# Attention probabilities transposed by the DMA engines as 16-bit planes instead of by TensorE

## The reference

```python
scores = scale * np.matmul(q_c, k_c.transpose(0, 1, 2, 4, 3))
scores = scores - np.max(scores, axis=-1, keepdims=True)
attn = np.exp(scores)
attn = attn / (np.sum(attn, axis=-1, keepdims=True) + 1e-09)
out = np.matmul(attn, v_c)
```

## Time and profile before

| | us |
|---|---|
| median of 3 runs (1153.63 to 1153.79) | 1153.75 |
| the profiled execution | 1154.12 |
| its span, first to last instruction | 1152.0 |
| PE busy | 1134.8 |
| ACT busy | 264.4 |
| DVE busy | 514.9 |

### The profile page before, as it was taken

The page is one execution under the profiler, slowest core; times in us unless marked ns, Lnnn a source line. Parts: engine busy times, 40 slices in busy tenths (PEclk is TensorE's granted clock), DMA queues, the critical chain, the costliest instruction groups (busy, mean ns, idle before and its releaser), DMA issues.

```text
span 1152.0 us, 19512 instructions
## 1 busy us (share of the span) xinstructions
PE 1134.8 (99%) x6790; PEld 998.3 (87%) x6791; DVE 514.9 (45%) x1142; ACT 264.4 (23%) x413; POOL 312.3 (27%) x191
## 2 busy tenths in 40 slices
PE   8999999999999999999999999999999999999995
PEld 5898889999999999999999998889987888888884
DVE  5454335222222222222223248888655555555553
ACT  3322232231111123111113211112333032032320
POOL 7300000060000006000002501100387686086680
PEclk8999999999999999999999999999999999999998
DMA  8221120330000012000002201101662662062630
GB/s 323 78 73 48 43 82 0 120 101 0 0 0 0 0 56 89 0 0 0 0 0 74 72 28 28 20 7 27 192 175 66 180 231 89 27 231 84 217 121 16
DMA packets 48881, 83.51 MB, mean 72 GB/s; under 512 B 8143, under 2 KB 32847, under 8 KB 48722
## 3 DMA queue, kind: packets, MB, share of 16 engines
q1 hardware_dynamic: 43922, 70.77, 19.4%
q0 software_dynamic: 4496, 11.56, 3.2%
q10 hardware_dynamic: 432, 0.79, 0.2%
HBM read 73.48 MB, written 10.92 MB: 73 GB/s over the span
## 4 chain that ended last, share of the span: by engine, by line
PE 98%; DMA 1%; DVE 0%; issue 0%; SPq 0%; ACT 0%; DVEq 0%
PE psum L1298 15%; PE psum L1300 15%; PE psum L1299 15%; PE psum L1332 12%; PE psum L1334 11%; PE psum L1333 11%; PE psum L1511 4%; PE psum L1513 4%; PE psum L1512 4%; PE psum L1495 2%; PE psum L1221 1%; PE psum L1472 1%; PE psum L1205 1%; PE psum L1213 1%; DMA qkT<-in_qk 1%; PE psum L1265 1%
## 5 line engine op out<-in xcount | busy, mean ns | idle before, releaser
L440 POOL TENSOR_TENSOR weights_r<-weights,weights_r 128x1024 fp32r<-128x1024 f32 x96 | 233.3, 2455 | 619.5 <-ACT weights_r L611 618.3
L1298 PE MATMUL psum<-xhi,weights_r 128*128 128x384 f32 x768 | 259.0, 337 | 0.3 <-DVEq L816 0.3
L1300 PE MATMUL psum<-xhi,weights_r 128*128 128x384 f32 x768 | 257.1, 335 | 0.0
L1299 PE MATMUL psum<-xlo,weights_r 128*128 128x384 f32 x768 | 256.9, 335 | 0.0
L1332 PE MATMUL psum<-weights_r,hhi 128*128 128x512 f32 x576 | 227.5, 395 | 0.0
L1334 PE MATMUL psum<-weights_r,hlo 128*128 128x512 f32 x576 | 224.9, 390 | 0.0
L1333 PE MATMUL psum<-weights_r,hhi 128*128 128x512 f32 x576 | 224.7, 390 | 0.0
L606 ACT ACTIVATE hhi<-psum 128x384 fp32r<-128x384 f32 x192 | 94.4, 492 | 489.9 <-PE psum L1300 489.9
L827 DVE SCALAR_TENSOR_TENSOR hlo<-psum,hhi 128x384 fp32r<-128x384 f32 x192 | 106.3, 556 | 220.0 <-ACT hhi L606 219.9
L1298 PEld LDWEIGHTS psum<-xhi,weights_r 128*128 128x128 f32 x768 | 144.2, 188 | 2.0 <-DVEq L816 0.8
L1299 PEld LDWEIGHTS psum<-xlo,weights_r 128*128 128x128 f32 x768 | 144.3, 188 | 0.9
(11 more groups left out here) (185 smaller groups left out, 1070.4 us busy)
## 6 DMA issues: line engine op xcount, KB each, us to landing
weights<-in_moe_w SPq DMA_DIRECT2D x96, 512.0 KB, 6.1
qkT<-in_qk SPq DMA_DIRECT2D x18, 512.0 KB, 3.8
x_rows<-xfin SPq DMA_DIRECT2D x18, 256.0 KB, 5.0
v_rows<-in_v SPq DMA_DIRECT2D x15, 256.0 KB, 2.8
wg_row<-in_gate_rows SPq DMA_DIRECT2D x1, 2048.0 KB, 7.4
v_rows<-in_v ACTq DMA_DIRECT2D x3, 256.0 KB, 6.3
meta<-slot_table SPq DMA_DIRECT2D x26, 1.0 KB, 2.1
rows<-x_rows,meta POOLq DMA_INDIRECT x26, 3.9
```

Of the source, the lines that this page charges most:

```text
L440: gp.tensor_tensor(rounded(set_, 1, c), raw(set_, c), rounded(set_, 0, c).bitcast(F32), ALU.subtract).then_inc(sem("w_lo"), 1)
L1298: mm(out_, ahi, bhi, start=(i == 0), stop=False)
L1299: mm(out_, ahi, blo, start=False, stop=False)
L1300: last = mm(out_, alo, bhi, start=False, stop=(i == n - 1))
```

## The change

Of the attention that is threaded through expert 0 (not of the first group's), the transposes leave PE. A probability is a 32-bit word. ACT copies the words of a tile (128 x 512) as 16-bit integers into two planes, first all low halves, then all high halves (split_planes, 128 x 1024 elements of 16 bits). SP issues one DMA transpose for the tile, which turns eight blocks of 128 x 128 halves. ACT then writes the halves of the transposed planes back next to each other into pT (join_planes), which attend reads as before. Each copy is one instruction.

The buffers lie in a part of acc that the first five groups don't write and in the place of gT. There are two, so tile 2 uses those of tile 0. The order on ACT becomes: step 4 split 0, step 5 split 1, step 6 join 0 and the exponential of tile 2, step 7 join 1 and split 2, step 8 x of tiles 0 and 1, step 10 join 2, step 12 x of tile 2. SP's loop is written out five times, and each transpose waits for its split between the reloads.

```diff
+            def transpose_planes(a, j):
+                sp.wait_ge(sem("planes_ready"), (a - 1) * TG + j + 1)
+                sp.dma_start_transpose(planes_T[j % 2][:, :, :].rearrange("p h (u t) -> p (h u) t", t=P),
+                                       planes[j % 2][:, :, :].rearrange("p h n -> p (h n)")).then_inc(planes_in[j % 2], 16)
+            def attention_loads(a, more=True):
+                if more:
+                    next_qk(a, 0)
+                    next_qk(a, 1)
+                transpose_planes(a, 0)
+                transpose_planes(a, 1)
+                if more:
+                    next_qk(a, 2)
+                transpose_planes(a, 2)
+                if more:
+                    for j in range(TG):
+                        next_v(a, j)
...
+            def split_planes(t, j):
+                act.wait_ge(sem("probs_ready"), t + 1)
+                words = probs[:, j, :, :, :].rearrange("p c r k -> p (c r k)").bitcast(U16)
+                sc.activation(planes[j % 2][:, :, :], words.rearrange("p (n h) -> p h n", h=2), ACT.Copy)\
+                    .then_inc(sem("planes_ready"), 1)
+            def join_planes(t, j, nth_in):
+                act.wait_ge(planes_in[j % 2], 16 * nth_in)
+                words = pT[:, j, :, :].rearrange("p u t -> p (u t)").bitcast(U16)
+                sc.activation(words.rearrange("p (n h) -> p h n", h=2), planes_T[j % 2][:, :, :], ACT.Copy)\
+                    .then_inc(sem("pT_ready"), 1)
...
+                if step == 4:
+                    split_planes(t0, 0)
                 if step == 5:
-                    take_pT(t0, 0, PT_B[0])
-                    take_pT(t0 + 1, 1, PT_B[1])
+                    split_planes(t0 + 1, 1)
+                if step == 6:
+                    join_planes(t0, 0, 2 * a - 1)
                     exponentials(t0 + 2, 2)
+                if step == 7:
+                    join_planes(t0 + 1, 1, a)
+                    split_planes(t0 + 2, 2)
                 if step == 10:
-                    take_pT(t0 + 2, 2, PT_B[2])
+                    join_planes(t0 + 2, 2, 2 * a)
...
                     score(2, S_B[2])
-                    transpose_p(t, 0, PT_B[0])
-                    transpose_p(t + 1, 1, PT_B[1])
...
-                if step == 10:
-                    pe.wait_ge(sem("x_ready"), t + 1)
-                    transpose_p(t + 2, 2, PT_B[2])
```

More of the change, by code:

```diff
@@ L12, in chunked_attention_then_two_moes @@
     F32, F32R, BF16 = mybir.dt.float32, mybir.dt.float32r, mybir.dt.bfloat16
-    I32, U32 = mybir.dt.int32, mybir.dt.uint32
+    I32, U32, U16 = mybir.dt.int32, mybir.dt.uint32, mybir.dt.uint16
     ALU = mybir.AluOpType
@@ L105, in chunked_attention_then_two_moes @@
     gT = tile("gT", [P, KT, P], F32, base)
+    over_gT = base
     base += 4 * KT * P
@@ L108, in chunked_attention_then_two_moes @@
     xTlo_r, _ = both("xTlo", [P, KT, P], at["acc"] + 4 * NB * D + 4 * F + 8 * D)
+    late = at["acc"] + 4 * (NT - TG) * D
+    planes = [tile(f"planes{i}", [P, 2, 2 * KT * C], U16, late + 8 * i * D) for i in range(2)]
+    planes_T = [tile(f"planes_T{i}", [P, 2, KT * P], U16, at_) for i, at_ in enumerate((late + 4 * D, over_gT))]
     rows0 = tile("rows0", [P, D], F32, gx)
@@ L188, in chunked_attention_then_two_moes @@
     S_B = [(4, 5), (6, 7), (5, 6)]
-    PT_B = [4, 7, 4]
     X_B = [(4, 5), (6, 7), (6, 7)]
@@ L229, in chunked_attention_then_two_moes @@
     v_in = [sem(f"v_in{i}") for i in range(TG)]
+    planes_in = [sem(f"planes_in{i}") for i in range(2)]
     raw_in = [[sem(f"raw_in{i}_{c}") for c in range(NW)] for i in range(2)]
@@ L327, in _ @@
                 next_v(0, j)
[L328 to L332, removed]
+            def transpose_planes(a, j):
[14 more added lines that the diff above has]
+                        next_v(a, j)
+            for a in range(1, NG):
+                attention_loads(a, more=(a < NG - 1))
             sp.wait_ge(sem("o_psum"), NT)
@@ L563, in take_first_x, with attention @@
                 sc.activation(by_pair(x[:, :, j * P:(j + 1) * P]), x_in(FIRST_B[j]), ACT.Copy).then_inc(sem("x_ready"), 1)
-            def attention(step, t0):
+            def attention(step, t0, a):
                 if step == 1:
@@ L629, in group @@
                     if t0 is not None:
-                        attention(f, t0)
+                        attention(f, t0, n + 1)
                     if first is not None and f == 2:
@@ L645, in group @@
                     for step in range(FT, 2 * FT):
-                        attention(step, t0)
+                        attention(step, t0, n + 1)
                     act.wait_ge(sem("x_ready"), t0 + TG)
```

## The result

| | before | after |
|---|---|---|
| median of 5 runs, us | 1153.79 (1153.63 to 1155.19) | 1147.87 (1147.39 to 1148.26) |
| profiled execution, us | 1154.12 | 1147.39 |
| its span, us | 1152.0 | 1145.4 |

The medians lie 5.9 us apart, where 4.8 were forecast. The ratio of the runs is 0.9947, with a 95% interval of 0.9936 to 0.9959.

What follows compares the result with a forecast made beforehand. TensorE, busy 1134.8 of 1152.0 us, was taken to bound the kernel. Removed transposes (-6.3 us) and five waits of 0.3 us summed to -4.8 us, forecasting 1149.0 us, range 1146.8 to 1175.

Steps and rivals of the forecast that it cites:

- The transposes: 60 transposes leave TensorE in five attention stretches: 0.82 us at step 5 and 0.44 at step 10, 6.3 us in all.
- Splits 1.06: Each ScalarE copy of a tile's halves into two planes takes 1.06 us, with ends of 0.53 and 2.1.
- Joins 1.06: Each ScalarE copy of transposed halves back into pT takes 1.06 us, with ends of 0.53 and 2.1.
- the slack: Everything queued behind join 0 on ScalarE has about 0.5 us before attend 0 is late.
- L = 4.6: Time from the end of a split to the landing of its DMA transpose, taken as 4.6 us.
- the packet row: Upper bound for the DMA transpose: 64 pieces per engine at 81 ns each are 5.2 us, L = 7.3.
- The wait of 0.3 us a stretch: TensorE waits 0.3 us for late planes in each of five stretches, because L = 4.6 exceeds 4.3.
- Everything else hidden: TensorE waits for nobody in the stretches before the change, so every wait the change adds is new.
- The sum: -6.3 us for the transposes plus 5 x 0.3 for the wait gives -4.8 us, a median of 1149.0 us.
- The rival of late planes: Join 0 blocks ScalarE's queue and attend 0 holds TensorE: 1162 us, 1177 with clock loss; chance 0.25.
- the point of no wait: Up to L = 4.3 us TensorE does not wait; beyond it each microsecond is a wait in each stretch.
- The third qk load: In SyncE's queue behind a wait for planes, it goes at 76.05 us, covered by over 25 us.

Runs made afterwards that it cites:

- e1: The kernel before without the 60 transposes and 15 copies into pT, nothing added, attend reading the first group's pT: 1159.32 us, 0.9947 of the kernel before.
- e0: The changed kernel run again, beside the kernel before at 1165.5 us: 1160.78 us, ratio 0.9953.
- e2: The changed kernel with the old transposes and copies into pT put back, joins written to an unread buffer: 1165.79 us against 1165.5 before, ratio 1.0000.
- e4: The changed kernel with split 1 moved from step 5 to step 6, ahead of join 0: 1158.82 us, 1.0039 of the kernel before.
- e5: The changed kernel with both splits moved to step 6, ahead of join 0: 1182.52 us, 1.0242 of the kernel before.
- e6: The changed kernel with one more dense ScalarE copy per stretch, behind join 2: 1149.09 us in one execution.

## Why the prediction was right

- **The transposes.** Forecast 1.26 us per stretch from the starts, 1.46 by the chain; measured 1.33. Between attend 0 and attend 2 the distance fell from 9.97 us to 9.47, so step 10 gave 0.50 where I had 0.44; the remaining 0.83 is step 5, where I had 0.82. e1 shows that the whole change of a stretch is this.
- **Splits 1.06:** measured 1.05. **Joins 1.06:** measured 1.37, the term whose price was off. It made the slack 0.1 to 0.2 us instead of 0.5, and nothing else.
- **L = 4.6:** measured 3.1 from issue, and the issue follows the split's end by 0.03 us (73.25 and 73.28). This is the term that was mis-sized most. The rows bracketed it (2.8 and 7.3) and I went to the packet row; the plain load of the same bytes, 2.8 to 3.0, was the nearer one. The wait of 0.3 us a stretch thus didn't come, 1.5 us in all. The Trainium skill, "DMA: Bandwidth & Descriptors", section "Latency and other measured facts", with its 261 GB/s had given an estimate of L = 3.1; the 0.6 us between 128 and 256 KB are 218 GB/s, near it. The Trainium skill, "VectorE: DVE Perf Modes", section "The three transpose paths", has 1309 ns for one block of 128 x 128; eight of them in a row, 10.5 us, are not what happens here, where eight land in 3.1 us.
- **Everything else hidden:** right in four stretches (e1, e2), wrong in the first. I had said that TensorE waits for nobody there, and read the cover only for the new waits, not for the old ones: the removed transposes had been hiding a wait for VectorE. It costs 0.73 us in the profile, so 5 x 1.33 = 6.7 became 5.9. In other executions it costs more where the clock falls behind it (e0).
- **The sum was helped by luck.** The forecast was 1.1 us short: 1.5 for the wait that didn't come and 0.35 for the transposes, less 0.73 for the wait that I had not seen. Two errors of opposite sign brought 4.8 nearer to 5.9 than the terms were.
- **The rival of late planes** did not happen, but its price was tested: e4 and e5 confirm one microsecond per microsecond and stretch, and the clock beyond it (1.6 us measured behind 1.9 us of pause, and 2.8 behind 4.1, where I had put 3). With the measured join the point of no wait lay at L = 4.0 to 4.1, not 4.3, and break-even about 5.4.
- The third qk load went at 76.64, not 76.05, because the second transpose is issued only when split 1 is over (75.34) and its issue of 1.24 us stands before the load; it was covered, as said.

## What to carry to other kernels

Where one engine is busy throughout and the others are idle, moving its work to a longer path is worth the removed stream time, provided that the path starts early enough; lay the new chain out instruction by instruction against the first consumer, and check both what becomes late and which old wait the removed work was covering. For a DMA not in the trace, the plain transfer of the same bytes was the nearest guess here. Such a schedule stands near a cliff: 0.1 to 0.2 us of slack here, and TensorE's pauses cost clock on top of themselves: those of 1.9 to 2.1 us in some cases, those of 3.0 to 4.3 us in every one seen. And a wait that ends at a moment set by another engine takes up whatever was gained before it: compare where the waits end, not how long they are.

## What the runs showed of the hardware

- A DMA transpose of 128 x 1024 16-bit elements from SBUF to SBUF lands 3.1 us after issue, one of 128 x 512 after 2.5; they take SyncE 1.24 and 1.27 us to issue, a plain load of 512 KB 0.34.
- ScalarE copies 1024 16-bit elements per partition in 1.03 us dense, 1.05 with a 4-byte stride read and 1.37 with a 4-byte stride written, whichever of two tiles it writes (e2, e6).
- After 1.9 us without work TensorE's granted clock fell to its lower level for most of 4 us in four of five stretches in one execution of e4; after 1.93 us in e1 and 2.06 us in e5 it stayed at 1.00, after 2.13 in e6 and 3.17 in e0 it fell; after 4.1 to 4.3 us it fell in every stretch of e5.
- With GpSimd busy, an eight-element VectorE instruction took from 0.7 to 2.3 us (1.20 in the profile shown) instead of 0.17, and ended 0.02 to 0.04 us after GpSimd's instruction in all twelve profiles; the reciprocal of the same size behind it took 0.20 us in either case. That the one holds up the other is my inference from these ends; no run takes GpSimd's work away.
